# The last pass of an up projection on 64 rows: two token halves side by side in TensorE's array

## The chip, the cores and the metric

The kernel runs on one core of a Trainium2 chip. The metric is the device time of one execution in microseconds. One execution was also recorded by the hardware profiler; its rows are used below. PE is TensorE, DVE is VectorE, ACT is ScalarE, POOL is GpSimd and SP is SyncE. PEld is the part of TensorE that loads the stationary operand.

## What is computed

Three layers follow each other on x of 2 x 4160 tokens with 192 channels. The first is a softmax-weighted sum over 7 past tokens. The other two are these:

```python
xk = mu_k * x + (1 - mu_k) * x_prev          # layer 2, x_prev is the token before
k = np.maximum(xk @ w_k, 0.0)                # up projection 1: 192 -> 1024
v = k * k @ w_v                              # down projection 1: 1024 -> 192
r = 1 / (1 + np.exp(-(xr @ w_r)))            # xr is mixed with mu_r
x = r * v
h = np.maximum(x @ w_in, 0.0)                # layer 3, up projection 2: 192 -> 1024
gate = sigmoid(3-tap convolution of h over the tokens, per channel)
out = (h * gate) @ w_out                     # down projection 2
```

The change touches the two up projections alone. Both sum over 192 channels, that is 128 and 64 rows of the array.

## The kernel before, in words

**Tiles.** The 8320 tokens lie on 128 partitions with 65 tokens each. They are worked off in NG = 13 groups of G = 5, so that one group has N = 640 columns of tokens, in two halves of HN = 320. The 1024 hidden channels are NC = 8 chunks of 128.

**One chunk of an up projection** (up_products, L311 to L321) is written to a PSUM tensor of two banks, one half of the tokens in each. Each operand is split into a rounded part (hi) and a rest (lo) of type float32r. Five terms are summed, each for both halves, so a chunk has ten matmuls of 320 columns:

- terms 1 to 3 use the first 128 channels: w_hi with a_hi, w_lo with a_hi, w_hi with a_lo;
- terms 4 and 5 use the last 64 channels. Their tile a2 (xk2_s or y2_s) holds the hi part in one half of the partitions and the lo part in the other, and w2_hi and w2_lo hold the same 64 rows of weights twice. So term 4 gives w2_hi times (hi + lo) in one matmul, and term 5 gives w2_lo times (hi + lo).

For x the hi part of the last channels lies in partitions 0 to 63, for y in 64 to 127.

**Order on TensorE.** It is written out by hand. phase_a(i) (L431) holds the eight chunks of up1 for group i+1, the ten transposes of y of group i, the gate matmuls r_unit of group i+1, and the five blocks of down2 for group i-1. phase_b(i) (L444) holds the eight chunks of up2 for group i, the five blocks of down1 for group i+1 and the ten transposes of the attention result for group i+2. A loop runs both for i = 1 to 10. A chunk writes one of two PSUM tensors, up[c % 2]; from the third chunk on it waits until ACT has read the chunk two before (k_ok or h_ok).

**ScalarE.** k_relu (L546) and h_relu (L567) read a finished chunk out of PSUM. x_hi (L520 to L528) and y_hi_part (L530 to L540) make the hi parts; part 2 of either writes the 64 rows of a2. VectorE makes the lo parts from them (x_lo, L811; y_lo_part, L828).

**VectorE.** In phase_b(i) it works through six windows of convolution and gate (L843 to L857) of group i, and between them mixes x for group i+2 (L781 to L803) and multiplies y of group i+1 (y_mult, L818). The transposes of y that open the next phase_a wait for the last y_mult. In phase_a it ends the windows and computes the attention sum (L740, L745).

Of the kernel before, what the change touches and what calls it, by code (L numbers as in the profile page):

```python
# [25 lines left out]
F32R = mybir.dt.float32r  # L26
ALU = mybir.AluOpType
ACT = mybir.ActivationFunctionType
AX_X = mybir.AxisListType.X

P = 128


def mixer_kernel(nc, x, weight_gen, mu_k, mu_r, w_k, w_v, w_r, w_in, conv_w, w_out, out):
# [4 lines left out]
    NC = F // P  # L39
    D2 = D - P  # L40
# [3 lines left out]
    NG = TPP // G  # L44
    N = G * P
    HN = N // 2
# [4 lines left out]
    BANK = 512  # L51
# [18 lines left out]
    with ctx:  # L70
        def sb(name, shape, dt=F32):
            return ctx.enter_context(nc.sbuf_tensor(name, shape, dt))

        def sem(name):
            return ctx.enter_context(nc.semaphore(name))


        wk_hi, wk_lo, wk2_hi, wk2_lo = [sb(n, [P, F], F32R) for n in ("wk_hi", "wk_lo", "wk2_hi", "wk2_lo")]
        wi_hi, wi_lo, wi2_hi, wi2_lo = [sb(n, [P, F], F32R) for n in ("wi_hi", "wi_lo", "wi2_hi", "wi2_lo")]
# [21 lines left out]
        xkr2 = sb("xkr2", [P, N])  # L101
        xk_hi = sb("xk_hi", [P, N], F32R)
        xk_lo = sb("xk_lo", [P, N], F32R)
        xk2_s = sb("xk2_s", [P, N], F32R)
# [2 lines left out]
        y_hi = sb("y_hi", [P, N], F32R)  # L107
        y_lo = sb("y_lo", [P, N], F32R)
        y2_s = sb("y2_s", [P, N], F32R)
        HW = N + 5 * P  # L110
        h = sb("h", [P, NC * HW])
        cv = [sb(f"cv{i}", [P, N]) for i in range(2)]
# [3 lines left out]
        up = [ctx.enter_context(nc.psum_tensor(f"up{i}", [P, 2 * BANK], F32)) for i in range(2)]  # L116
        mid = ctx.enter_context(nc.psum_tensor("mid", [P, 2 * BANK], F32))
# [20 lines left out]
        x_used, at_step, at_sum, at_ok = [sem(n) for n in ("x_used", "at_step", "at_sum", "at_ok")]  # L138
        t_done, xt_ok, xt_free = [sem(n) for n in ("t_done", "xt_ok", "xt_free")]
        mix, xk_ok, xr_ok, x2_ok = [sem(n) for n in ("mix", "xk_ok", "xr_ok", "x2_ok")]  # L140
        xhi_ok, xlo_ok = sem("xhi_ok"), sem("xlo_ok")
        u1_done, k_ok, ksq_ok = [sem(n) for n in ("u1_done", "k_ok", "ksq_ok")]
        r_done, sg_ok, d_done, y_ok = [sem(n) for n in ("r_done", "sg_ok", "d_done", "y_ok")]
        yt_done, yhi_ok, ylo_ok = [sem(n) for n in ("yt_done", "yhi_ok", "ylo_ok")]
        u2_done, h_ok, h_free = [sem(n) for n in ("u2_done", "h_ok", "h_free")]
# [12 lines left out]
        def eq(g, n):  # L158
            return isinstance(g, int) and g == n
# [24 lines left out]
        def y_parts(g):  # L184

            return (xk_hi, xk_lo, xk2_s) if eq(g, NG - 1) else (y_hi, y_lo, y2_s)
# [64 lines left out]
        def _(pool):  # L251
# [16 lines left out]
            pool.wait_ge(h_ok, NC)  # L268
            nc.gpsimd.tensor_copy(h3[:, :, HW - 2 * P:HW], h3[:, :, 2 * P:4 * P]).then_inc(h_keep, 1)
            for g in range(3, NG):  # L270
# [4 lines left out]
        def _(pe):  # L275
# [32 lines left out]
                    pe.wait_ge(ylo_ok, 2 * g + 1)  # L308
                    transposes(mid, y, D, range(G), D2, yt_done)

            def up_products(dst, c, w_hi, w_lo, w2_hi, w2_lo, a_hi, a_lo, a2, done, part_ready):  # L311
                cols = slice(c * P, (c + 1) * P)
                terms = ((w_hi, a_hi), (w_lo, a_hi), (w_hi, a_lo), (w2_hi, a2), (w2_lo, a2))
                for t, (w, a) in enumerate(terms):
                    if part_ready is not None:
                        part_ready(t)
                    for half in range(2):
                        mm = nc.tensor.matmul(dst[:, half * BANK:half * BANK + HN], w[:, cols],  # L318
                                              a[:, half * HN:(half + 1) * HN],
                                              start=(t == 0), stop=(t == len(terms) - 1))  # L320
                mm.then_inc(done, 1)  # L321

            def up1(g, c):
                ready = None
                if c == 0:
                    def ready(t):
                        if t == 0:
                            pe.wait_ge(xhi_ok, 2 * g + 1)
                        elif t == 2:
                            pe.wait_ge(xlo_ok, 2 * g + 1)  # L330
                        elif t == 3:
                            pe.wait_ge(xhi_ok, 2 * g + 2)
                            pe.wait_ge(xlo_ok, 2 * g + 2)
                if c >= 2:
                    pe.wait_ge(k_ok, NC * g + c - 1)
                elif eq(g, 1):
                    pe.wait_ge(k_ok, NC - 1 + c)
                elif not eq(g, 0):
                    pe.wait_ge(h_ok, NC * g - NC - 1 + c)
                up_products(up[c % 2], c, wk_hi, wk_lo, wk2_hi, wk2_lo, xk_hi, xk_lo, xk2_s, u1_done, ready)  # L340

            def up2(g, c):
                ready = None
                if c == 0:
                    def ready(t):
                        if t == 0:
                            pe.wait_ge(yhi_ok, 2 * g + 1)
                        elif t == 2:
                            pe.wait_ge(ylo_ok, 2 * g + 1)
                        elif t == 3:  # L350
                            pe.wait_ge(yhi_ok, 2 * g + 2)
                            pe.wait_ge(ylo_ok, 2 * g + 2)
                if c >= 2:
                    pe.wait_ge(h_ok, NC * g + c - 1)
                elif eq(g, NG - 1):
                    pe.wait_ge(h_ok, NC * g - 1 + c)
                else:
                    pe.wait_ge(k_ok, NC * g + 2 * NC - 1 + c)
                up_products(up[c % 2], c, wi_hi, wi_lo, wi2_hi, wi2_lo, *y_parts(g), u2_done, ready)

            def r_unit(g, u):
                if u == 0:
# [13 lines left out]
            def down_block(dst, n, lhs, b, w, chunk_ready):  # L376
                for c in range(NC):
                    if chunk_ready is not None:
                        chunk_ready(c)
                    mm = nc.tensor.matmul(dst[:, n * D:(n + 1) * D], lhs[:, c, b * P:(b + 1) * P], w[:, c, :],  # L380
                                          start=(c == 0), stop=(c == NC - 1))
                return mm
# [48 lines left out]
            def phase_a(i, with_y=True, with_out=True):  # L431
                for c in range(NC):
                    up1(i + 1, c)
                    if with_y and c in (0, 2):
                        yt_part(i, c // 2 + 1)
                    if 3 <= c <= 5:
                        r_unit(i + 1, c - 3)
                    if with_out and c >= 5:
                        down2(i - 1, c - 5)
                if with_out:  # L440
                    down2(i - 1, G - 2)
                    down2(i - 1, G - 1)
# [51 lines left out]
            for n in range(2):  # L494
                def ready(c):
                    pe.wait_ge(g_ok, NC * NG + c + 1)
                mm = down_block(dn[0], n, gat3, n, wo_sb, ready if n == 0 else None)
# [4 lines left out]
        def _(act):  # L502
# [6 lines left out]
            def halves(v):  # L509
                return v.rearrange("p (s n) -> p s n", s=2)  # L510
# [9 lines left out]
            def x_hi(g, part):  # L520
                if part == 1:
                    if not eq(g, 0):
                        act.wait_ge(u1_done, NC * g)
                    act.wait_ge(xk_ok, g + 1)
                    nc.scalar.activation(xk_hi[:, :], xk1[:, :], ACT.Copy).then_inc(xhi_ok, 1)  # L525
                else:
                    act.wait_ge(x2_ok, g + 1)
                    nc.scalar.activation(xk2_s[0:D2, :], xkr2[0:D2, :], ACT.Copy).then_inc(xhi_ok, 1)  # L528

            def y_hi_part(g, part):  # L530
                hi, _, y2 = y_parts(g)
                act.wait_ge(yt_done, 2 * g + part)
                if part == 1:
                    if eq(g, NG - 1):
                        act.wait_ge(u1_done, NC * NG)
                    elif not eq(g, 0):
                        act.wait_ge(u2_done, NC * g)
                    nc.scalar.activation(hi[:, :], mid[:, 0:N], ACT.Copy).then_inc(yhi_ok, 1)
                else:
                    nc.scalar.activation(y2[D2:P, :], mid[D2:P, 0:N], ACT.Copy).then_inc(yhi_ok, 1)  # L540

            def k_relu(g, c):
                act.wait_ge(u1_done, NC * g + c + 1)
                if c == 0 and not eq(g, 0):
                    act.wait_ge(d_done, 3 * g)
                nc.scalar.activation(halves(ksq3[:, c, :]), up3[c % 2], ACT.Relu).then_inc(k_ok, 1)  # L546
# [10 lines left out]
                nc.scalar.activation(y[:, lo * D:hi * D], dn[u % 2][:, 0:(hi - lo) * D], ACT.Sigmoid).then_inc(sg_ok, 1)  # L557

            def h_relu(g, c):
                act.wait_ge(u2_done, NC * g + c + 1)  # L560
                if eq(g, 0):
                    pass
                else:
                    act.wait_ge(h_free, NC * g - NC + c + 1)
                    if eq(g, 1) and c == 0:
                        act.wait_ge(h_keep, 1)
                nc.scalar.activation(halves(h3[:, c, 2 * P:2 * P + N]), up3[c % 2], ACT.Relu).then_inc(h_ok, 1)  # L567
# [499 lines left out]
```

## Time and profile before

| | |
|---|---|
| median of 3 runs | 789.57 us (788.32 to 791.07) |
| span of the profiled execution | 788.2 us |
| its own time | not listed apart from the runs above; the fastest of them lies 0.1 us over the span, the median 1.4 us |
| PE busy | 731.6 us, 93% |
| PEld busy | 724.4 us, 92% |
| DVE busy | 653.0 us, 83% |
| ACT busy | 427.1 us, 54% |
| POOL busy | 11.8 us, 1% |

A row of a group of instructions shows the line, the engine, the operation, the tiles out<-in, the shape and the count, then the busy time and the mean duration of one. Matmuls overlap, so the busy time over the count is shorter than the mean duration: the first is the pace, the second the time from entering the array until the modelled end. "128*128" is the part of the array, rows by columns, that the instruction uses.

### The profile page before, as it was taken

How to read it: one execution, taken by the hardware profiler on the slowest of the kernel's cores; microseconds unless marked ns; L12 is line 12 of the kernel's file. 1: busy time of each engine (PE TensorE's matmuls, PEld its weight loads, DVE VectorE, ACT ScalarE, POOL GpSimd, SP SyncE). 2: the span in 40 equal slices, each digit the busy share in tenths (PEclk: the TensorE clock that was granted, in tenths of full speed). 3: DMA queues.
4: the chain of work that ended last, by engine and by line, in shares of the span. 5: the costliest groups of instructions: out<-in, count | busy, mean ns of one | idle time of the engine just before them, and what ended most of it. 6: DMA issues, size and time to landing. Idle time of an engine off the chain costs nothing.

```text
span 788.2 us, 12723 instructions
## 1 busy us (share of the span) xinstructions
PE 731.6 (93%) x4715; PEld 724.4 (92%) x4715; DVE 653.0 (83%) x834; ACT 427.1 (54%) x726; POOL 11.8 (1%) x21
## 2 busy tenths in 40 slices
PE   0199898999999999999999999999999999999898
PEld 0189898999999999999999999999999999999798
DVE  5898899799999899699697896996996996905794
ACT  1064746457457356366464473473563564655783
POOL 1000000000000000000000000000000000000000
PEclk9999999999999999999999999999999999999999
DMA  9501010020100200200200201102002000000001
GB/s 253 152 7 61 1 61 0 4 73 1 68 17 0 85 0 0 85 0 0 85 0 0 85 0 39 46 0 85 0 0 85 0 0 25 0 1 26 1 22 39
DMA packets 7831, 27.71 MB, mean 35 GB/s; under 512 B 940, under 2 KB 3716, under 8 KB 6274
## 3 DMA queue, kind: packets, MB, share of 16 engines
q1 hardware_dynamic: 7506, 26.39, 10.1%
q10 hardware_dynamic: 304, 1.05, 0.5%
q8 instruction: 12, 0.20, 0.1%
q14 instruction: 9, 0.07, 0.0%
HBM read 21.05 MB, written 6.39 MB: 35 GB/s over the span
## 4 chain that ended last, share of the span: by engine, by line
PE 49%; DVE 33%; issue 12%; ACT 3%; DMA 1%; DVEq 1%; SPq 0%; ACTq 0%
PE dn L380 23%; PE up L318 19%; DVE cv L846 8%; DVE gat L857 5%; DVE cv L843 4%; DVE prod L740 3%; PE dn L372 2%; PE dn L373 2%; DVE att L745 2%; PE mid L278 2%; DVE y L818 2%; DVE xk_s L811 1%; DMA xin<-in_x 1%; DVE cv L849 1%; ACT h L567 1%
## 5 line engine op out<-in xcount | busy, mean ns | idle before, releaser
L380 PE MATMUL dn<-wv_sb,ksq 128*128 128x192 f32 x1040 | 179.2, 326 | 0.0
L380 PEld LDWEIGHTS dn<-wv_sb,ksq 128*128 128x128 f32 x1040 | 169.7, 190 | 0.1
L380 PE MATMUL dn<-wo_sb,gat 128*128 128x192 f32 x992 | 167.0, 326 | 0.0
L380 PEld LDWEIGHTS dn<-wo_sb,gat 128*128 128x128 f32 x992 | 161.7, 190 | 0.0
L567 ACT ACTIVATE h<-up 128x640 f32<-128x640 f32 x104 | 73.1, 704 | 116.6 <-PE up L318 116.5
L546 ACT ACTIVATE ksq<-up 128x640 f32<-128x640 f32 x104 | 72.9, 701 | 67.6 <-PE up L318 65.7
L846 DVE SCALAR_TENSOR_TENSOR cv<-h,prm,cv 128x640 f32<-128x640 f32 x96 | 85.0, 886 | 26.9 <-ACT cv L590 23.8
L740 DVE TENSOR_TENSOR prod<-xin,wgt 128x960 f32<-128x960 f32 (+1 forms) x78 | 90.3, 1171 | 4.8
L843 DVE TENSOR_SCALAR cv<-h,prm 128x640 f32<-128x640 f32 x88 | 48.2, 548 | 55.3 <-ACT h L567 54.1
L745 DVE TENSOR_TENSOR att<-att,prod 128x960 f32<-128x960 f32 (+1 forms) x78 | 91.1, 1169 | 0.9
L572 ACT ACTIVATE cv<-cv 128x640 f32<-128x640 f32 (+1 forms) x100 | 72.2, 722 | 35.8 <-DVE cv L849 32.8
L849 DVE SCALAR_TENSOR_TENSOR cv<-h,prm,cv 128x640 f32<-128x640 f32 x96 | 86.5, 901 | 3.4
L857 DVE TENSOR_TENSOR gat<-h,cv 128x640 f32<-128x640 f32 x92 | 75.3, 819 | 0.3
L550 ACT ACTIVATE ksq<-ksq 128x640 f32<-128x640 f32 x104 | 74.9, 734 | 0.0
L318 PE MATMUL up<-xk_hi,wk_hi 128*128 128x320 f32 x208 | 57.4, 357 | 0.8 <-ACT xk_hi L525 0.8
L318 PE MATMUL up<-y_hi,wi_hi 128*128 128x320 f32 x192 | 52.7, 355 | 0.0
L318 PE MATMUL up<-xk_s,wk_hi 128*128 128x320 f32 x208 | 48.2, 313 | 2.5 <-DVE xk_s L811 2.5
L318 PE MATMUL up<-xk_lo,wk_hi 128*128 128x320 f32 x208 | 48.4, 314 | 0.0
L318 PE MATMUL up<-xk_hi,wk_lo 128*128 128x320 f32 x208 | 48.4, 314 | 0.0
L318 PE MATMUL up<-xk_s,wk_lo 128*128 128x320 f32 x208 | 47.9, 312 | 0.0
L601 ACT ACTIVATE o_sb<-dn 128x384 f32<-128x384 f32 (+1 forms) x39 | 16.9, 432 | 56.8 <-PE dn L380 56.8
L518 ACT ACTIVATE xt<-mid 128x640 f32<-128x640 f32 (+1 forms) x26 | 18.5, 712 | 53.3 <-PE mid L278 53.0
(119 smaller groups left out, 1112.2 us busy)
## 6 DMA issues: line engine op xcount, KB each, us to landing
xin<-in_x SPq DMA_DIRECT2D x11, 1152.0 KB, 5.4
out<-o_sb SPq DMA_DIRECT2D x12, 480.0 KB, 2.7
wgt<-in_weight_gen SPq DMA_DIRECT2D x1, 1680.0 KB, 12.0
xin<-in_x SPq DMA_DIRECT2D x1, 960.0 KB, 4.5
wv_sb<-in_moe_w_v SPq DMA_DIRECT2D x1, 768.0 KB, 12.8
wo_sb<-in_moe_w_out SPq DMA_DIRECT2D x1, 768.0 KB, 8.7
gat<-in_moe_w_k ACTq DMA_DIRECT2D x1, 512.0 KB, 4.9
gat<-in_moe_w_k ACTq DMA_DIRECT2D x2, 256.0 KB, 6.9
```

The source lines that it names most:

```text
L318: mm = nc.tensor.matmul(dst[:, half * BANK:half * BANK + HN], w[:, cols], a[:, half * HN:(half + 1) * HN], start=(t == 0), stop=(t == len( ...
L380: mm = nc.tensor.matmul(dst[:, n * D:(n + 1) * D], lhs[:, c, b * P:(b + 1) * P], w[:, c, :], start=(c == 0), stop=(c == NC - 1))
L546: nc.scalar.activation(halves(ksq3[:, c, :]), up3[c % 2], ACT.Relu).then_inc(k_ok, 1)
L550: nc.scalar.activation(ksq3[:, c, :], ksq3[:, c, :], ACT.Square).then_inc(ksq_ok, 1)
L567: nc.scalar.activation(halves(h3[:, c, 2 * P:2 * P + N]), up3[c % 2], ACT.Relu).then_inc(h_ok, 1)
L572: nc.scalar.activation(tile[:, 0:width], tile[:, 0:width], ACT.Sigmoid).then_inc(gs_ok, 1)
L740: nc.vector.tensor_tensor(v, x_tap(k), w_tap(k), ALU.mult)\
L745: nc.vector.tensor_tensor(acc, acc, term(k), ALU.add)\
L843: nc.vector.tensor_scalar(o[:, :], h3[:, c, P:P + N], taps[1], None, ALU.mult).then_inc(tap, 1)
L846: nc.vector.scalar_tensor_tensor(o[:, :], h3[:, c, 0:N], taps[0], o[:, :], ALU.mult, ALU.add).then_inc(tap, 1)
L849: nc.vector.scalar_tensor_tensor(o[:, :], h3[:, c, 2 * P:2 * P + N], taps[2], o[:, :], ALU.mult, ALU.add).then_inc(cv_ok, 1)
L857: nc.vector.tensor_tensor(dst[:, c, :], h3[:, c, P:P + N], conv_tile(w, c)[:, :], ALU.mult).then_inc(g_ok, 1)
```

## The change

Term 5 no longer takes all 128 rows. It multiplies w2_lo with the hi part alone, 64 rows, so the product of the two lo parts is left out. The lower half of the tokens runs in one half of the array's rows, the upper half of the tokens in the other half of the rows, each into its own bank. For that the hi part of one token half must also lie in the other 64 partitions: a new tile xy2_o takes it, by one more copy on ACT ahead of the old one in x_hi part 2 and in y_hi_part part 2. Each of the two last matmuls increments the semaphore, so the counts that ScalarE waits for are doubled.

```diff
+        xy2_o = sb("xy2_o", [P, HN], F32R)
...
-                terms = ((w_hi, a_hi), (w_lo, a_hi), (w_hi, a_lo), (w2_hi, a2), (w2_lo, a2))
+                terms = ((w_hi, a_hi), (w_lo, a_hi), (w_hi, a_lo), (w2_hi, a2))
...
                     for half in range(2):
                         mm = nc.tensor.matmul(dst[:, half * BANK:half * BANK + HN], w[:, cols],
                                               a[:, half * HN:(half + 1) * HN],
-                                              start=(t == 0), stop=(t == len(terms) - 1))
-                mm.then_inc(done, 1)
+                                              start=(t == 0), stop=False)
+
+                nc.tensor.matmul(dst[:, 0:HN], w2_lo[0:D2, cols], lower, start=False, stop=True).then_inc(done, 1)
+                nc.tensor.matmul(dst[:, BANK:BANK + HN], w2_lo[D2:P, cols], upper,
+                                 start=False, stop=True).then_inc(done, 1)
...
                             pe.wait_ge(xhi_ok, 2 * g + 2)
+                            pe.wait_ge(xo_ok, g + 1)
...
-                up_products(up[c % 2], c, wk_hi, wk_lo, wk2_hi, wk2_lo, xk_hi, xk_lo, xk2_s, u1_done, ready)
+                up_products(up[c % 2], c, wk_hi, wk_lo, wk2_hi, wk2_lo, xk_hi, xk_lo, xk2_s,
+                            xk2_s[0:D2, 0:HN], xy2_o[D2:P, :], u1_done, ready)
...
-                up_products(up[c % 2], c, wi_hi, wi_lo, wi2_hi, wi2_lo, *y_parts(g), u2_done, ready)
+                up_products(up[c % 2], c, wi_hi, wi_lo, wi2_hi, wi2_lo, *y_parts(g),
+                            xy2_o[0:D2, :], y_parts(g)[2][D2:P, HN:N], u2_done, ready)
...
                     act.wait_ge(x2_ok, g + 1)
+                    nc.scalar.activation(xy2_o[D2:P, :], xkr2[0:D2, HN:N], ACT.Copy).then_inc(xo_ok, 1)
                     nc.scalar.activation(xk2_s[0:D2, :], xkr2[0:D2, :], ACT.Copy).then_inc(xhi_ok, 1)
...
+                    if eq(g, NG - 1):
+                        act.wait_ge(u2_done, 2 * NC * g)
+                    nc.scalar.activation(xy2_o[0:D2, :], mid[D2:P, 0:HN], ACT.Copy).then_inc(yo_ok, 1)
                     nc.scalar.activation(y2[D2:P, :], mid[D2:P, 0:N], ACT.Copy).then_inc(yhi_ok, 1)
...
-                act.wait_ge(u1_done, NC * g + c + 1)
+                act.wait_ge(u1_done, 2 * (NC * g + c + 1))
...
-                act.wait_ge(u2_done, NC * g + c + 1)
+                act.wait_ge(u2_done, 2 * (NC * g + c + 1))
```

## Rows read from the trace of the kernel before

**Rows 1.** Stretches: length, busy time of PE, PEld, DVE, ACT, POOL, then PEclk.

```profile
0.00:75.96 75.96, 37.55 (x220) 35.72 (x221) 58.01 (x72) 25.41 (x36) 4.33 (x9) 1.00 0.43 122
75.96:129.00 53.04, 45.48 (x287) 44.69 (x287) 48.59 (x63) 30.48 (x49) 2.63 (x2) 0.96 0.07 23
129.00:683.49 554.49, 551.55 (x3596) 548.47 (x3596) 485.20 (x612) 307.03 (x525) 4.79 (x10) 1.00 0.08 28
683.49:738.00 54.51, 53.77 (x351) 53.49 (x350) 23.95 (x31) 32.02 (x55) 0.00 (x0) 1.00 0.03 10
738.00:788.20 50.20, 43.25 (x266) 42.01 (x266) 37.30 (x60) 32.13 (x64) 0.00 (x0) 1.00 0.07 25
```

**Rows 2.** The two stretches of one period, in the same columns.

```profile
435.01:461.13 26.12, 25.83 (x170) 25.53 (x170) 24.56 (x37) 13.57 (x23) 0.00 (x0) 1.00 0.17 63
461.13:490.42 29.29, 29.29 (x192) 29.29 (x193) 22.62 (x24) 16.43 (x30) 0.45 (x1) 1.00 0.00 1
```

**Rows 3.** The chain that ended last, pieces of that period: start, length, what.

```profile
433.53 1.48 PE up L318 x10
435.12 0.71 ACT h L567
435.95 0.56 DVE cv L843
...
459.91 0.82 DVE gat L857
460.73 0.28 DVE y L818
461.01 0.12 issue
461.13 0.76 PE mid L278 x5
461.89 0.15 PE up L318
```

**Rows 4.** Waits: engine and line, what for, us in total, times, longest.

```profile
PE mid L278 <- DVE y L818: 5.9, 10, 3.1
DVE cv L843 <- ACT h L567: 54.1, 9, 6.7
```

**Rows 5.** Groups of matmuls and of loads: busy us, mean ns of one.

```profile
L318 PE MATMUL up<-xk_s,wk_lo 128*128 128x320 f32 x208 | 47.9, 312 | 0.0
L318 PE MATMUL up<-y_s,wi_lo 128*128 128x320 f32 x192 | 43.9, 310 | 0.0
L318 PEld LDWEIGHTS up<-y_s,wi_lo 128*128 128x128 f32 x192 | 32.4, 189 | 0.0
```

**Rows 6.** Timeline inside a run of up chunks: start, busy length, engine.

```profile
403.20 0.46 PE L318 MATMUL up<-y_s,wi_hi 128*128 128x320 f32 x2
403.35 0.34 PEld L318 LDWEIGHTS up<-y_s,wi_lo 128*128 128x128 f32 x2
403.49 0.46 PE L318 MATMUL up<-y_s,wi_lo 128*128 128x320 f32 x2
403.79 0.45 PE L318 MATMUL up<-xk_hi,wk_hi 128*128 128x320 f32 x2
```

**Rows 7.** Timeline where the array had stood idle: two loads, their matmuls.

```profile
739.92 0.30 PEld L318 LDWEIGHTS up<-xk_s,wi_hi 128*128 128x128 f32 x2 [2.92 <-ACT xk_s L540]
```

**Rows 8.** Timeline of ACT and DVE around the second half of y.

```profile
411.12 0.70 ACT L540 ACTIVATE y_s<-mid 64x640 fp32r<-64x640 f32 x1
412.52 0.40 ACT L594 ACTIVATE h<-h 128x256 f32<-128x256 f32 x1
412.61 0.82 DVE L828 TENSOR_TENSOR y_s<-mid,y_s 64x640 fp32r<-64x640 f32 x1
```

**Rows 9.** Timeline of ACT and DVE around the second half of x.

```profile
41.38 0.74 ACT L528 ACTIVATE xk_s<-xkr 64x640 fp32r<-64x640 f32 x1 [1.58 <-DVE xkr L793]
42.15 0.82 DVE L811 TENSOR_TENSOR xk_s<-xkr,xk_s 64x640 fp32r<-64x640 f32 x1 [0.67 <-ACT xk_s L528]
...
451.42 0.72 ACT L528 ACTIVATE xk_s<-xkr 64x640 fp32r<-64x640 f32 x1
...
456.29 0.82 DVE L811 TENSOR_TENSOR xk_s<-xkr,xk_s 64x640 fp32r<-64x640 f32 x1
```

More of the change, by code:

```diff
@@ L140, in mixer_kernel @@
         mix, xk_ok, xr_ok, x2_ok = [sem(n) for n in ("mix", "xk_ok", "xr_ok", "x2_ok")]
-        xhi_ok, xlo_ok = sem("xhi_ok"), sem("xlo_ok")
+        xhi_ok, xlo_ok, xo_ok, yo_ok = [sem(n) for n in ("xhi_ok", "xlo_ok", "xo_ok", "yo_ok")]
         u1_done, k_ok, ksq_ok = [sem(n) for n in ("u1_done", "k_ok", "ksq_ok")]
@@ L309, in yt_part, with up_products @@
                     transposes(mid, y, D, range(G), D2, yt_done)
-            def up_products(dst, c, w_hi, w_lo, w2_hi, w2_lo, a_hi, a_lo, a2, done, part_ready):
+            def up_products(dst, c, w_hi, w_lo, w2_hi, w2_lo, a_hi, a_lo, a2, lower, upper, done, part_ready):
                 cols = slice(c * P, (c + 1) * P)
-                terms = ((w_hi, a_hi), (w_lo, a_hi), (w_hi, a_lo), (w2_hi, a2), (w2_lo, a2))
+                terms = ((w_hi, a_hi), (w_lo, a_hi), (w_hi, a_lo), (w2_hi, a2))
                 for t, (w, a) in enumerate(terms):
@@ L351, in ready @@
                             pe.wait_ge(yhi_ok, 2 * g + 2)
+                            pe.wait_ge(yo_ok, g + 1)
                             pe.wait_ge(ylo_ok, 2 * g + 2)
@@ L522, in x_hi @@
                     if not eq(g, 0):
-                        act.wait_ge(u1_done, NC * g)
+                        act.wait_ge(u1_done, 2 * NC * g)
                     act.wait_ge(xk_ok, g + 1)
@@ L534, in y_hi_part @@
                     if eq(g, NG - 1):
-                        act.wait_ge(u1_done, NC * NG)
+                        act.wait_ge(u1_done, 2 * NC * NG)
                     elif not eq(g, 0):
-                        act.wait_ge(u2_done, NC * g)
+                        act.wait_ge(u2_done, 2 * NC * g)
                     nc.scalar.activation(hi[:, :], mid[:, 0:N], ACT.Copy).then_inc(yhi_ok, 1)
                 else:
+                    if eq(g, NG - 1):
+                        act.wait_ge(u2_done, 2 * NC * g)
+                    nc.scalar.activation(xy2_o[0:D2, :], mid[D2:P, 0:HN], ACT.Copy).then_inc(yo_ok, 1)
                     nc.scalar.activation(y2[D2:P, :], mid[D2:P, 0:N], ACT.Copy).then_inc(yhi_ok, 1)
             def k_relu(g, c):
-                act.wait_ge(u1_done, NC * g + c + 1)
+                act.wait_ge(u1_done, 2 * (NC * g + c + 1))
                 if c == 0 and not eq(g, 0):
```

## The prediction

> **What bounds the kernel now.** I read the stretches of the span first. The loop of ten periods fills 129 to 683 us, and in it TensorE is busy 551.6 of 554.5 us at the full clock (PEclk 1.00, the upper of its two levels, 2.4 GHz), VectorE 485 and ScalarE 307 [rows 1]. So TensorE sets the pace of 70% of the span. But one period of 55.4 us has two parts, and the chain of waits shows that they differ [rows 2, 3]. From the transposes of y to the end of the first up2 chunk (29.3 us, the next phase A) the chain stays on TensorE, and VectorE has 6.7 us to spare ahead of its first window [rows 4]. From there to the last y_mult (26.1 us, phase B) the chain is VectorE's own, one instruction behind the other, 24.6 us busy; TensorE then stands for the last y_mult before it can transpose. The summed wait is 5.9 us in ten times, of which one, at the start, is 3.1, so about 0.3 a period [rows 4]; together with the issue of the first transpose I take 0.4. Phase B is thus held by two engines at once: a faster TensorE gains nothing there, a slower one costs all but those 0.4 us.
>
> Then the up chunks. Two 320-column matmuls of a term begin 0.29 us after the two before (403.20, 403.49, 403.79), so one enters every 147 ns, while each lasts about 308 ns by itself: a pair shows 0.455 us, less 0.147 [rows 6]; the group means are 310 and 312 [rows 5]. The array thus always holds two matmuls, the next one entering 161 ns (308 less 147) before the last one has left. A load starts with the matmul before its own and is hidden. Where the array stood idle, two loads show 0.30 us against 0.33 to 0.34 in the stream [rows 6, 7]; one load lasts 0.19 [rows 5], so a second load follows an idle start after about 0.11, which I take as what one load needs.
>
> **The change, part by part.** There are 13 x 8 x 2 = 208 chunks.
>
> Removed: two matmuls of 147 ns a chunk, 294 ns. Added: two matmuls of 64 rows, still 320 columns each. If they run beside each other they take the time of one, 147 ns, so the gain that is asked for is 147 ns a chunk.
>
> The change-over. Before, no matmul of 64 rows stands in the stream, so this price has no row and is bounded. In the eight matmuls ahead of the pair every result is the sum over all 128 rows; in the pair the lower and the upper rows must deliver separate sums to separate banks. With the old matmul still 161 ns inside, its last columns need the rows joined while the first of the pair need them apart. From below: nothing, as for the hand-over from one term to the next [rows 6], which changes only operands. From above, for the matmuls alone: each change-over lets the array empty, 161 ns, and there are two a chunk, into the pair and out of it. I take the upper value, because the reason why neighbours can overlap in rows 6 (all use the same joined rows) is the one the edit takes away, so the nearest row is that of one whole matmul, 308 ns. A chunk then costs 2 x 161 - 147 = 175 ns more.
>
> The Trainium skill states the same (TensorEngine Tiling (Array Packing), Key Properties: "Changing tiling mode (not just tile) drains the TensorE"). No run here shows it yet; it would also speak for the upper value.
>
> The two loads. The pair needs two loads as before. If the second begins only with the first of the pair, as each load begins with the matmul ahead of it now [rows 6], its matmul comes 108 ns late (0.30 less 0.19, rounded) and a chunk costs 283 ns more. If in addition neither load can run ahead of a change-over, two more loads of 108 ns lie open, 499 ns. I take none of these, since the two loads go to different rows, and keep both for the range.
>
> The copies. A copy of 256 columns takes 0.40 us and one of 640 takes 0.70 to 0.72, so one of 320 about 0.46 [rows 8, 9]; 26 of them are 12 us more on an engine that is busy 54%. In the loop the x half ends at 452.1 and its reader starts at 456.3, so 4 us cover it [rows 9]; without them the price would be 0.46 a period. The y half ends at 411.82 and its reader starts at 412.61: 0.79 against 0.46, still covered [rows 8]; what follows on ACT there is 0.46 later, and the next chunk's readers have waits to spare. At the start nothing covers it: VectorE waits for ACT and TensorE for VectorE (41.38, 42.15), 0.46 us [rows 9]. Near the end, for group 12, TensorE stands 2.9 us on the same two steps, 0.46 more [rows 7]. Together 0.9 us. The new semaphore waits belong to copies that are done before the lo parts, so nothing queues for them; the second increment costs nothing, since the reader waited for the later matmul before too.
>
> **The sum.** Of the 208 chunks, 80 lie in the phase A part of the ten periods, 16 in the start (first phase A and the one of 76 to 90 us) and 16 from 683 to 738 us, all in stretches where TensorE is busy end to end: 112. Another 80 lie in phase B of the ten periods, less 0.4 us a period. The remaining 16 (phase B of group 0, and up2 of group 12) stand among waits for VectorE and ScalarE (PE busy 45.5 of 53.0 us and 43.3 of 50.2 [rows 1]) and are costed at nothing; covered so, they would cost 2.8 us if that cover were gone. 192 x 0.175 = 33.6, less 10 x 0.4 = 4.0, plus 0.9: 30.5 us. On the profiled span of 788.2 that is 818.7. The median of the runs lies 1.4 us over this span, so the forecast is **820 us**.
>
> **The rivals.**
>
> (1) *Faster: no emptying.* The pair runs side by side and the change-over is free, as between terms. The gain is up to 147 ns a chunk; if the second load waits for the first of the pair, 108 ns late, it is 39. Phase B gives nothing, for VectorE holds it. 112 x 0.147 = 16.5 less 0.9 is 15.6: 774 us. With 39 ns: 4.4 less 0.9, 786 us. Middle: 780. For it: all hand-overs in the trace, between terms and between shapes, are seamless. Against it: none of them parts the rows. It decides from below 73 ns a change-over, half of 147.
>
> The skill (TensorE: Matmul & The Clock Gate, Part 3) tells of row tiles that start some 4 ns apart. That would bear out the 147 ns inside the pair; it says nothing of neighbours that use all rows, and no row here shows it.
>
> (2) *Same: the pair is not a pair.* The second of the 64-row matmuls follows the first after 147 ns, because of one stream of operands or of a load that needs as long in the stream as the matmul does (0.33 for two, 0.147 apart [rows 6]). Then ten matmuls stay ten, and with 0.9 us of copies it is 790.5 us. For it: a load and its matmul keep the same pace in the stream throughout. Against it: one load needs only 0.11 [rows 7].
>
> (3) *Much slower: the loads lie open too.* 192 x 0.283 - 3.1 is 51 us, 841; with 499 ns, 93 us, 882. It has the same sign as my forecast and fills the range upward.
>
> **How the numbers follow.** About 0.3% (2.4 us) is what a measurement here can tell from no change. Slower: 0.54, of which an incomplete emptying (some 795 to 815) 0.12, the forecast 0.24, open loads 0.18. Faster (rival 1): 0.33, some of it near 786. Same (rival 2, and gains and costs that cancel): 0.13. The range runs from 775, which leaves out only the perfect pair, to 862, half way between the two cases of open loads: about 0.08 below, 0.1 above. The likeliest case has 812 to 845 for itself.
>
> **What would show it.** By my forecast the profile after shows a period of 55.4 + 16 x 0.175 - 0.4 = 57.8 us; in a chunk the first matmul of 64 rows starts 0.31 us (not 0.147) after the last of 128 rows, the second within 0.02 us of it, and the next chunk's first 0.31 us after that. A chunk in a run of chunks takes 1.65 us, not 1.47. VectorE's wait for h grows in phase B. If the starts stand 0.147 apart all the way but the pair's two coincide, rival 1 is right, the chunk is 1.32 us and TensorE's wait for the last y_mult grows from 0.4 to about 1.6 us a period, so that only phase A shortens. If the pair's two matmuls are 0.147 apart, it is rival 2. The copies are wrong if TensorE waits for xy2_o in the loop. The forecast fails as a whole if the period stays at or under 55.4 us.

## The result and the profile after

The changed kernel takes 831.07 us (median of 4 runs, 830.75 to 832.39) against 789.65 us: slower by a ratio of 1.053, with a 95% interval of 1.0514 to 1.0546. The profiled execution spans 829.1 us, 40.9 more than the one before. The forecast was 820 us, with a range of 775 to 862.

The stretches of the span, for the same stages as in [rows 1], though not cut at exactly the same instructions. Columns: length, busy time of PE, PEld, DVE, ACT and POOL, PEclk, DMA share, GB/s.

```profile
0.00:79.30 79.30, 40.83 (x213) 35.45 (x214) 57.30 (x71) 25.80 (x37) 4.34 (x9) 1.00 0.40 117
79.30:134.60 55.30, 51.54 (x308) 44.52 (x306) 49.97 (x65) 32.92 (x53) 3.06 (x2) 0.97 0.07 22
134.60:718.53 583.93, 583.93 (x3575) 527.98 (x3575) 486.14 (x611) 314.27 (x543) 4.56 (x10) 1.00 0.07 26
718.53:771.00 52.47, 52.47 (x322) 47.96 (x320) 19.92 (x26) 27.88 (x48) 0.00 (x0) 1.00 0.03 10
771.00:829.10 58.10, 51.62 (x304) 46.98 (x302) 40.59 (x64) 38.84 (x74) 0.00 (x0) 0.97 0.06 21
```

VectorE does the same work as before; the clock is at its upper level in the loop, as it was before but for 3.4 us of the first period (127.9 to 131.3). What has changed is that TensorE shows no idle time at all in the loop, while its weight loads cover less of it.

In the start the clock differs as well. Two matmuls of 320 columns have a record of 0.73 us while the clock is at its lower level, and of 0.46 us at the upper one [rows 6]. The kernel before leaves the lower level at 46.0 us, the changed kernel at 50.9 (the PEclk column has no value for the time before that and shows 1.00):

```profile
45.39 0.73 PE L318 MATMUL up<-xk_lo,wk_hi 128*128 128x320 f32 x2
48.27 0.73 PE L321 MATMUL up<-xk_lo,wk_hi 128*128 128x320 f32 x2
```

The two parts of a period, to be held against [rows 2]:

```profile
455.76:483.44 27.68, 27.68 (x170) 24.83 (x171) 26.07 (x39) 13.91 (x24) 0.00 (x0) 1.00 0.16 57
483.44:514.53 31.09, 31.09 (x193) 28.29 (x192) 21.18 (x22) 17.02 (x32) 0.46 (x1) 1.00 0.01 3
```

A period is 58.77 us, not 55.42. Phase B grew by 1.56 us and phase A by 1.80. Now the chain of waits in phase B, which was VectorE's own in [rows 3], stays on TensorE (start, length, what):

```profile
478.57 1.17 PE up L321 x8
479.74 0.34 PE up L325
480.08 0.00 PE up L326
480.08 1.37 PE up L321 x8
481.45 0.34 PE up L325
481.79 0.00 PE up L326
481.80 1.37 PE up L321 x8
```

One chunk that follows another takes 1.37 + 0.34 = 1.71 to 1.72 us, where ten matmuls took 1.47: 0.248 us more, from the starts of single instructions. TensorE no longer stands for y_mult in the loop, and VectorE's wait for h has grown (from 6.7 in [rows 4], longest wait last):

```profile
PEld up L325 <- issue: 40.9, 208, 0.3
DVE cv L857 <- ACT h L581: 71.9, 10, 8.8
```

The first of these rows is new. In all 208 chunks the loading part of TensorE stands still ahead of the 64-row load, 40.9 / 208 = 0.197 us each. This is counted from the end of the load before, so it shows where TensorE stands and not yet what that costs. The timeline of one chunk shows where (start, busy length, engine):

```profile
430.08 0.46 PE L321 MATMUL up<-xk_s,wk_hi 128*128 128x320 f32 x2
430.46 0.18 PEld L325 LDWEIGHTS up<-xk_s,wk_lo 64*128 64x128 f32 x1 [0.19 <-issue]
430.46 0.41 PE L325 MATMUL up<-xk_s,wk_lo 64*128 64x320 f32 x1
430.46 0.18 PEld L326 LDWEIGHTS up<-xy_o,wk_lo 64*128 64x128 f32 x1
430.47 0.41 PE L326 MATMUL up<-xy_o,wk_lo 64*128 64x320 f32 x1
430.81 0.30 PEld L382 LDWEIGHTS dn<-wr_sb,xr 128*128 128x128 f32 x2 [0.16 <-issue]
430.81 0.59 PE L382 MATMUL dn<-wr_sb,xr 128*128 128x192 f32 x2
```

(L382 is the gate block that follows this chunk.) The last 128-row matmul starts 0.147 after 430.08, at 430.22. The 64-row load starts at 430.46: 0.24 later, or 0.09 beyond the slot of 0.147. It is not hidden either: the record of its matmul is 0.41 long instead of 0.31, because it waits 0.10 for its own weights. Both matmuls of the pair do start together, 3 to 4 ns apart in all 208 pairs. On the way out it is the same: the load for the next 128-row matmul starts at 430.81, 0.24 after the pair's real start at 430.57 (the start of its record and the 0.10 for the load), and its matmul waits 0.108 for it, seen from the next load (0.30 for two loads less 0.19). Each change-over thus costs 0.09 of standing still and 0.10 to 0.11 for an open load, some 0.198 us; two of them less the 0.147 that the pair saves are the 0.248 us. I call the 0.09 emptying. The record of the last 128-row matmul, whose end is modelled, lasts 0.31 us: the next matmul starts behind that end (0.345 after it), but its load starts before it (0.24), so what exactly the load waits for the trace does not show.

```profile
L325 PE MATMUL up<-xk_s,wk_lo 64*128 64x320 f32 x104 | 43.3, 417 | 0.0
L326 PE MATMUL up<-xy_o,wk_lo 64*128 64x320 f32 x104 | 43.3, 416 | 0.0
```

These are the groups in the place of L318 with wk_lo in [rows 5]: a mean of 417 ns instead of 312, the difference being the open load.

### The profile page after: what moved, and what is told of

It reads as the page before. It is cut to its first block, busy times and chain, and to the rows that moved or that the text cites. A ratio compares the mean times of both kernels' runs of the same rounds, so it can differ in the third digit from the quotient of the medians.

```text
span 829.1 us, 12750 instructions
## 1 busy us (share of the span) xinstructions
PE 780.4 (94%) x4715; PEld 702.9 (85%) x4715; DVE 653.9 (79%) x834; ACT 439.7 (53%) x752; POOL 12.0 (1%) x21
## 4 chain that ended last, share of the span: by engine, by line
PE 87%; DVE 8%; issue 2%; ACT 1%; DMA 1%; SPq 0%; DVEq 0%; ACTq 0%
PE dn L390 41%; PE up L321 29%; PE up L325 8%; PE mid L281 4%; PE dn L382 3%; PE dn L383 2%; DVE prod L754 2%; DVE att L759 1%; DMA xin<-in_x 1%; DVE cv L860 1%; DVE cv L857 1%; DVE gat L871 0%; DVE cv L863 0%; DVE wk_lo L959 0%; DVE att L754 0%
## 5 line engine op out<-in xcount | busy, mean ns | idle before, releaser
L390 PE MATMUL dn<-wv_sb,ksq 128*128 128x192 f32 x1040 | 185.4, 332 | 0.0
L390 PEld LDWEIGHTS dn<-wv_sb,ksq 128*128 128x128 f32 x1040 | 167.3, 190 | 9.6 <-issue 9.6
L390 PE MATMUL dn<-wo_sb,gat 128*128 128x192 f32 x992 | 169.6, 329 | 0.0
L860 DVE SCALAR_TENSOR_TENSOR cv<-h,prm,cv 128x640 f32<-128x640 f32 x96 | 84.9, 885 | 29.4 <-ACT cv L604 26.2
L863 DVE SCALAR_TENSOR_TENSOR cv<-h,prm,cv 128x640 f32<-128x640 f32 x96 | 84.9, 885 | 3.4
L321 PE MATMUL up<-xk_hi,wk_hi 128*128 128x320 f32 x208 | 60.6, 373 | 0.8 <-ACT xk_hi L535 0.8
L321 PE MATMUL up<-y_hi,wi_hi 128*128 128x320 f32 x192 | 55.1, 369 | 0.0
L528 ACT ACTIVATE xt<-mid 128x640 f32<-128x640 f32 (+1 forms) x26 | 18.5, 713 | 58.9 <-PE mid L281 58.8
L321 PE MATMUL up<-y_hi,wi_lo 128*128 128x320 f32 x192 | 44.1, 311 | 0.0
```

What stands on the lines that cost most here:

```text
L860: nc.vector.scalar_tensor_tensor(o[:, :], h3[:, c, 0:N], taps[0], o[:, :], ALU.mult, ALU.add).then_inc(tap, 1)
L863: nc.vector.scalar_tensor_tensor(o[:, :], h3[:, c, 2 * P:2 * P + N], taps[2], o[:, :], ALU.mult, ALU.add).then_inc(cv_ok, 1)
```

## The experiments

Nine kernels were run. The theory was the one just read: a change between 128-row and 64-row matmuls costs about 198 ns each way, and the pair itself is worth one slot. The rivals lay in the copies, in the 64-row matmuls themselves, in the number of rows, and in how much of a gain phase B would have let through.

**All but the matmuls.**

```diff
-                nc.tensor.matmul(dst[:, 0:HN], w2_lo[0:D2, cols], lower, start=False, stop=True).then_inc(done, 1)
-                nc.tensor.matmul(dst[:, BANK:BANK + HN], w2_lo[D2:P, cols], upper,
-                                 start=False, stop=True).then_inc(done, 1)
+                for half in range(2):
+                    nc.tensor.matmul(dst[:, half * BANK:half * BANK + HN], w2_lo[:, cols],
+                                     a2[:, half * HN:(half + 1) * HN],
+                                     start=False, stop=True).then_inc(done, 1)
```

> All of the change but its matmuls: the new tile, the 26 copies on ACT, the waits and the doubled increments, while term 5 stays two matmuls on all 128 rows. Theory (the cost is in TensorE's change-overs): 790.5 us, that is 0.9 over the kernel before, from the start and from group 12. Rival (the copies or the extra increments delay the readers of each chunk): a good part of the 41 us, over 800.

Measured 792.50 us, ratio 1.0037 (1.0023 to 1.0051) to a median of 789.32: 3.2 us, not 0.9. The rival is out, but the copies had been priced too low. The wait for the second half of x in the second group and the transposes of y behind it, before and in this kernel, then two more starts of these transposes:

```profile
74.43 0.54 PE L318 MATMUL up<-xk_s,wk_hi 128*128 128x320 f32 x2 [0.53 <-DVE xk_s L811]
75.19 0.76 PE L278 MATMUL mid<-ident,y 128*128 128x128 f32 x5
75.91 0.54 PE L321 MATMUL up<-xk_s,wk_hi 128*128 128x320 f32 x2 [1.02 <-DVE xk_s L826]
76.67 0.77 PE L281 MATMUL mid<-ident,y 128*128 128x128 f32 x5
463.35 0.65 PE L281 MATMUL mid<-ident,y 128*128 128x128 f32 x4 [0.29 <-DVE y L833]
518.85 0.76 PE L281 MATMUL mid<-ident,y 128*128 128x128 f32 x5 [0.28 <-DVE y L833]
```

The start has taken 1.5 us. The copy lies open twice in it, 0.49 us each time: for the first group, as was forecast, and again for the second, where the wait goes from 0.53 to 1.02. Of the other 0.5 us, 0.2 are a DMA that landed later, and the rest goes with a clock that left its lower level at 47.6 us instead of 46.0. The period is 55.50 against 55.42, 0.8 us over the ten, and the end is 0.5 us longer, as forecast. Why a period of which the copies are not on the chain is 0.08 longer was not followed up.

**Nine matmuls: the price of a free pair.**

```diff
-                    for half in range(2):
+                    for half in range(1 if t == 4 else 2):
...
-                                              start=(t == 0), stop=(t == len(terms) - 1))
+                                              start=(t == 0), stop=(t == (3 if half else 4)))
```

> The kernel before with the second matmul of term 5 left out (w2_lo is not applied to the upper token half), so nine matmuls of 128 rows a chunk: what a free pair would give. Theory (VectorE holds phase B, so that only 112 chunks pay): 789.7 less 112 x 0.147 = 773. Rival (all 208 chunks pay): 759.

Measured 780.50 us, ratio 0.9885 (0.9869 to 0.9902): 8.8 us less, neither 30.6 nor 16.5. The period is 54.64 us, 0.78 shorter, with these parts:

```profile
401.93:430.70 28.77, 28.64 (x185) 28.35 (x186) 22.63 (x24) 16.46 (x31) 0.45 (x1) 1.00 0.01 3
430.70:456.57 25.87, 24.42 (x161) 24.11 (x160) 24.55 (x37) 13.65 (x23) 0.00 (x0) 1.00 0.18 61
```

The cut at 430.70 lies 0.25 us further into its chunk than the one in [rows 2]; counted from the start of that chunk, phase A is 0.77 us shorter than before and phase B as long as before. Phase B is held as foretold: VectorE is busy 24.55 us there, as in [rows 2], and the wait for the last y_mult grows to about 1.5 us a period:

```profile
456.57 0.65 PE L278 MATMUL mid<-ident,y 128*128 128x128 f32 x4 [1.45 <-DVE y L818]
```

But phase A does not give its 8 x 0.147 = 1.18 us either. TensorE stands 0.4 us once a period ahead of down2. The sigmoid and the first load of down2, before and here:

```profile
416.37 0.50 ACT L557 ACTIVATE y<-dn 128x384 f32<-128x384 f32 x1
417.28 2.63 PEld L380 LDWEIGHTS dn<-wo_sb,gat 128*128 128x128 f32 x16
412.60 0.50 ACT L557 ACTIVATE y<-dn 128x384 f32<-128x384 f32 x1
413.23 0.95 PEld L380 LDWEIGHTS dn<-wo_sb,gat 128*128 128x128 f32 x6 [0.42 <-issue]
```

down2 takes a bank that ScalarE's sigmoid must have read (L410). The sigmoid ends at 413.10 and down2 follows at 413.23. Before, it ended at 416.87, 0.4 us ahead of the load. With TensorE faster, ScalarE's order of work in phase A is the next bound. The chunks of the start and the end gave less than their slots too: about 2 us, where 32 chunks at 0.147 had been counted as 4.7.

**One row half for both.** Both 64-row matmuls read the rows that hold the hi part; the sums stay those of the changed kernel.

```diff
...
-                nc.tensor.matmul(dst[:, 0:HN], w2_lo[0:D2, cols], lower, start=False, stop=True).then_inc(done, 1)
-                nc.tensor.matmul(dst[:, BANK:BANK + HN], w2_lo[D2:P, cols], upper,
+                nc.tensor.matmul(dst[:, 0:HN], w2_lo[rows, cols], lower, start=False, stop=True).then_inc(done, 1)
+                nc.tensor.matmul(dst[:, BANK:BANK + HN], w2_lo[rows, cols], upper,
...
-                            xk2_s[0:D2, 0:HN], xy2_o[D2:P, :], u1_done, ready)
+                            slice(0, D2), xk2_s[0:D2, 0:HN], xk2_s[0:D2, HN:N], u1_done, ready)
...
```

> The change with both matmuls of 64 rows in the same half of the rows, one token half after the other (the same sums as in the changed kernel). Theory (the pair in the changed kernel does run side by side, and the loss is in the two change-overs): one more slot of 147 ns in 192 chunks, 831 + 28 = 859 us. If the pair gained nothing from standing side by side: 831. If the price was that of two row halves being used together: near 790.

Measured 873.64 us (865.05 to 874.32), ratio 1.1031 (1.0973 to 1.1089). The period is 61.06 us, 2.29 more than in the changed kernel, or 16 x 0.143: the two follow each other, and the pair in the changed kernel did save its slot. Only the first of them pays for the open load:

```profile
L325 PE MATMUL up<-xk_s,wk_lo 64*128 64x320 f32 x104 | 43.8, 421 | 0.0
L326 PE MATMUL up<-xk_s,wk_lo 64*128 64x320 f32 x104 | 32.2, 310 | 0.0
```

It took 14.6 us more than the 859 that were expected, and most of that is a matter of the clock. The start is at the lower level until 59.0 us instead of 50.9, and the transposes of y first begin 5.2 us later than in the changed kernel, where eight more slots are 1.2. The other part lies near the end and is told in the last section.

**96 rows.**

```diff
+                    k = 96 if t == 4 else P
...
-                        mm = nc.tensor.matmul(dst[:, half * BANK:half * BANK + HN], w[:, cols],
-                                              a[:, half * HN:(half + 1) * HN],
+                        mm = nc.tensor.matmul(dst[:, half * BANK:half * BANK + HN], w[0:k, cols],
+                                              a[0:k, half * HN:(half + 1) * HN],
```

> The kernel before with term 5 on the first 96 of the 128 rows, for both token halves (part of the lo products and, for y, half of the hi products of w2_lo are left out). Theory (what counts is how the array is parted, and 96 rows leave it whole): 789.7 us, starts 147 ns apart. Rival (any change of the number of rows empties the array): ten slots and two change-overs of 198 ns, 192 x 0.396 less 4, about 861 us.

Measured 790.09 us, ratio 1.0008 (0.9998 to 1.0018). The group takes what it took with 128 rows (47.9 us and 312 ns in [rows 5]):

```profile
L319 PE MATMUL up<-xk_s,wk_lo 96*128 96x320 f32 x208 | 48.4, 314 | 0.0
```

So 96 rows among matmuls of 128 cost nothing. 96 rows are more than one half of the array and 64 are not; where between 64 and 96 the price begins was not tried.

**The two apart.**

```diff
...
+                        if t == 3 and half == 0:
+                            nc.tensor.matmul(dst[:, 0:HN], w2_lo[0:D2, cols], lower,
+                                             start=False, stop=True).then_inc(done, 1)
...
-                nc.tensor.matmul(dst[:, 0:HN], w2_lo[0:D2, cols], lower, start=False, stop=True).then_inc(done, 1)
```

> The changed kernel with its two matmuls of 64 rows apart: the one of the lower token half stands between the two matmuls of term 4, the other at the end. Four change-overs a chunk in place of two, and no pair. Theory (198 ns a change-over: 93 for emptying and 105 for a load that cannot run ahead): ten slots and four change-overs, 0.792 us more a chunk than before, 192 x 0.792 less 3, about 938 us. Rival (the price belongs to the 64-row matmuls themselves, not to the change of neighbours): no more than one slot over the changed kernel, 859.

Measured 952.40 us, ratio 1.2084 (1.2061 to 1.2106). The rival is out by 93 us; the theory's 938 was 14 us too low, again with a clock that stayed low longer, until 59.3 us at the start and for 27.3 us near the end. The period is 67.37 us, 11.95 over the kernel before; with the 0.4 us of cover that is 16 x 0.77, or 0.19 for each of the four change-overs. The loads stand still ahead of either:

```profile
PEld up L325 <- issue: 41.4, 208, 0.3
PEld up L328 <- issue: 33.7, 208, 0.3
```

**The pair twice.**

```diff
+                nc.tensor.matmul(dst[:, 0:HN], w2_lo[0:D2, cols], lower, start=False, stop=False)
+                nc.tensor.matmul(dst[:, BANK:BANK + HN], w2_lo[D2:P, cols], upper, start=False, stop=False)
```

> The changed kernel with the pair issued twice in a row (the product with w2_lo is added twice). Theory (two change-overs as before, and inside the 64-row part the loads run ahead again): one more slot of 147 ns in 192 chunks, 831 + 28 = 859 us. If loads stay open inside the 64-row part, 0.255 us a chunk: 880. If the second pair cannot overlap the first at all, 0.35 us a chunk: 898.

Measured 859.52 us, ratio 1.0896 (1.0878 to 1.0914), on the 859 of the theory. A second pair costs one slot, and its loads are hidden: the wait ahead of the first pair is 40.9 us as before, the second pair has none and the plain duration.

```profile
L326 PE MATMUL up<-xy_o,wk_lo 64*128 64x320 f32 x104 | 43.1, 415 | 0.0
L328 PE MATMUL up<-xy_o,wk_lo 64*128 64x320 f32 x104 | 32.0, 308 | 0.0
```

**Two pairs of neighbouring chunks side by side, and its control.** In phase A and phase B up(c) and up(c + 1) follow each other directly for even c, and what stood between them comes after. With pairs, the second chunk begins with its pair; the control has the same order and 128 rows throughout.

```diff
-                for c in range(NC):
-                    up1(i + 1, c)
...
+                for d in range(0, NC, 2):
+                    up1(i + 1, d)
+                    up1(i + 1, d + 1, True)
+                    for c in (d, d + 1):
...
+                if pair_first:
+                    nc.tensor.matmul(dst[:, 0:HN], w2_lo[0:D2, cols], lower, start=True, stop=False)
+                    nc.tensor.matmul(dst[:, BANK:BANK + HN], w2_lo[D2:P, cols], upper, start=True, stop=False)
```

> The changed kernel with two chunks brought together in phase A and phase B: the first ends with its pair, the second begins with its pair, so two pairs stand side by side and half of the change-overs go (all but the 16 chunks of up2 for groups 11 and 12). Theory (198 ns a change-over): a chunk costs 51 ns more than before, not 248. Phase B hides that in its 0.4 us, phase A does not: 789.7 + 104 x 0.051 + 8 x 0.248 + 0.9 is about 798 us. If the price were in the pairs, it would stay at 831.

> Control for the one with adjacent chunks: the kernel before with the same order of chunks, blocks and transposes, and all matmuls on 128 rows. Expected 789.7 us within 2 us by every theory; what it differs is the price of the order alone.

The control took 803.36 us (ratio 1.018, 1.0163 to 1.0197), so its expectation missed: the order costs 14.5 us by itself. With it the 798 us for the pairs missed as well. The second of two neighbouring chunks waits for ScalarE to empty its PSUM tensor:

```profile
PEld up L318 <- ACT ksq L550: 16.6, 24, 1.4
PE up L318 <- ACT ksq L550: 11.4, 12, 1.2
```

The kernel with pairs took 817.42 us (ratio 1.0368, 1.0351 to 1.0386), 14.1 over the control, where the change as it was made is 41.4 over its own. Per period it is 57.53 against 56.68 us, 0.85 or 16 x 0.053, and 51 ns a chunk were expected. The expectation had let phase B hide its half; here it does not, for in the control TensorE's wait for y_mult is already gone but for once (1.3 us). Half of the change-overs gone is most of the loss gone. Two pairs next to each other (start, busy length):

```profile
434.39 0.41 PE L332 MATMUL up<-xk_s,wk_lo 64*128 64x320 f32 x1
434.39 0.41 PE L333 MATMUL up<-xy_o,wk_lo 64*128 64x320 f32 x1
434.64 0.31 PE L318 MATMUL up<-xk_s,wk_lo 64*128 64x320 f32 x1
434.64 0.31 PE L319 MATMUL up<-xy_o,wk_lo 64*128 64x320 f32 x1
434.88 0.56 PE L324 MATMUL up<-xk_hi,wk_hi 128*128 128x320 f32 x2
```

**64 rows elsewhere.** The last test leaves the up projections alone and takes 64 rows in the gate blocks, in float32, without pair or copy.

```diff
-                    mm = nc.tensor.matmul(o, xkr2[:, b * P:(b + 1) * P], wr_sb[:, 1, :], start=False, stop=True)
+                    mm = nc.tensor.matmul(o, xkr2[D2:P, b * P:(b + 1) * P], wr_sb[D2:P, 1, :], start=False, stop=True)
```

> The kernel before with the second matmul of every gate block (r_unit, L373) on the 64 rows that hold its operand, in place of all 128 with zeros in the other 64; the sums are the same, the up projections are untouched. 65 blocks, each with a change-over in and one out. Theory (198 ns a change-over, for float32 as for float32r, with no pair and no copy about): 65 x 0.396 = 25.7 us in phase A, where TensorE sets the pace: about 815 us. Rival (the price belongs to two row halves used together or to the up chunks): 789.5.

Measured 813.36 us, ratio 1.0314 (1.0296 to 1.0333): 24.3 us for 65 blocks, 0.374 for the two change-overs of each. So neither a pair nor the copies are needed for the price. The zeros in the other 64 rows, which look like waste, are worth that much.

```profile
L373 PE MATMUL dn<-wr_sb,xkr 64*128 64x192 f32 x130 | 38.3, 375 | 0.0
PEld dn L373 <- issue: 14.6, 65, 0.2
```

No version tried beats the kernel before; only nine matmuls a chunk do, and they leave out a part that the others compute.

## Why the prediction was right, and where its terms were off

- **The bound.** Right. A slower TensorE costs in both phases; phase B gave back only the wait for y_mult, and the chain there moved from VectorE to TensorE. By the chunk's price the period should grow 16 x 0.248 less the 0.4 of cover, 3.6 us; it grew 3.35. The difference closes from the starts of the chunks. The cover was 0.51: before, the last chunk of the period takes 1.92 us (459.21 to 461.13) to the first load of the transposes and 0.06 more for that load, where a chunk takes 1.47. And the two chunks of a period that stand ahead of the transposes of y cost 0.05 less each, since the open load of a transpose is 0.06 long and not 0.11.
- **The pair.** Right: its two matmuls start together, and one row half for both costs 16 x 0.143 more a period. The Trainium skill (TensorE: Matmul & The Clock Gate, Part 3) lets matmuls on different row tiles start about 4 ns apart, and the trace agrees: 3 to 4 ns.
- **The change-over.** Right in kind, under-sized in amount; this is the term of the sum that failed. The Trainium skill (TensorEngine Tiling (Array Packing), Key Properties) says that a change of tiling mode drains TensorE. The trace above agrees as far as it reaches: the next matmul starts after the modelled end of the last one (0.345 against 0.31). The forecast took the whole remaining 161 ns for emptying and nothing for loads. Measured are 0.09 for emptying, since the next load starts 0.24 after the start of the last matmul and not 0.31, and 0.10 to 0.11 for a load that does not run ahead. The argument for leaving the loads out, that the two go to different rows, was wrong for what matters: they do not wait for each other, but the first load behind a change-over starts only 0.24 after the last matmul, whatever rows it goes to. 192 x (0.248 - 0.175) is 14 us too little.
- **The copies.** 0.9 was taken, 3.2 measured with all else as before. A copy of 320 columns took the 0.46 us that were taken (0.43 to 0.47), but at the start it lay open twice and not once, and the loop was not free.
- **The sum.** With both terms put right it would have been 30.5 + 14 + 2.3 = 47 us against 41.4 measured. The profiled spans, cut at the first transposes of y of each group, show where the rest went. The ten periods grew 32.4 us, not 160 x 0.248 - 4 = 35.7: 2.2 us by the 0.22 a period of the first point, and about 1 because the kernel before had its 3.4 us of low clock in the first of them. The start, up to these ten, grew 3.4 us, where 16 chunks and the copies come to 5.5: between 79 and 130 us nothing grew (50.97 us against 51.70), so the change-overs of the chunks that the forecast had counted there as open were covered, while the clock that stayed low until 50.9 us cost more (an estimate: half of 4.9, 2.4 us). The end grew 5.1 us. Errors of opposite sign, 16 us of terms put too low against 5 of cover put too low, made the forecast of 820 look closer than its parts were; that is luck.
- **Rival 1.** Out: the change-over is not free. Its price was wrong as well. The 16.5 us of gain would have been 8.8. A second bound, ScalarE's sigmoid ahead of down2, had only 0.4 us to spare and took 0.4 us of the gain in each period, and the chunks outside the ten periods gave about half of their slots.
- **Rivals 2 and 3.** The pair is a pair, and the second load does not wait for the first matmul. Open loads there are, but on top of a shorter emptying, so 0.248 a chunk and not 0.283 or 0.499.
- **The profile after.** Foretold were a period of 57.8 and a chunk of 1.65 us; they are 58.8 and 1.72.

## What to carry to other kernels

Before some matmuls of a stream are put on half of the rows, count the change-overs: here each costs 0.19 to 0.20 us, and a pair of 320 columns saves 0.147. By these numbers at least three pairs would have to stand together before the change pays; that is an estimate, and two were the most that was tried. Filling the idle rows of a matmul with zeros keeps the stream whole: in the gate blocks it is 24.3 us faster than leaving them out. Where two engines share the pace, price a gain by taking the work out for once: nine matmuls showed 8.8 us where the sum of slots said 30.6 and the best reading of the phases 16.5.

## What the runs showed that had not been expected

A matmul on 96 rows runs in the 128-row stream at the same pace, and one on 64 rows does not, alone or in a pair. The prediction had nothing on this; the theory behind the run had.

The load ahead of a change-over starts 0.24 us after the last matmul. In the kernel before, 4510 of the 4715 loads start within 5 ns of the start of a matmul.

The clock reached its upper level in the start at different times: at 46.0 us before and 50.9 in the changed kernel, at 59.0 and 59.3 in the kernels with one row half for both and with the two apart, but at 47.7 with the pair twice. Each kernel has the trace of one execution only, and no rule can be read from that.

Near the end of the kernels with one row half for both and with the two apart the granted clock fell to its lower level of 1.2 GHz for a long stretch: 23.9 us (from 813.4) in the one with one row half for both, 27.3 us (from 885.3) in the one with the two apart. It is the stage of up2 for the last group. In both TensorE had just stood 3.0 us for the lo part of y, which VectorE makes. Such a wait stands in the kernel before too [rows 7], without a fall of the clock, so it is not the cause by itself, and the cause stays open. The wait of the first kernel, then the stretches, first of the one, then of the other:

```profile
812.88 0.54 PE L321 MATMUL up<-xk_s,wi_hi 128*128 128x320 f32 x2 [2.99 <-DVE xk_s L843]
820.00:870.00 50.00, 49.05 (x244) 45.09 (x244) 31.25 (x52) 27.22 (x55) 0.00 (x0) 0.83 0.05 20
```

```profile
870.00:952.00 82.00, 72.35 (x334) 60.90 (x332) 44.31 (x69) 39.41 (x76) 0.00 (x0) 0.83 0.04 15
```

In the changed kernel PEclk is 0.97 in that stage. One of the four runs of the kernel with one row half took 865.05 us and the others 873.5 to 874.3. Its mean granted clock was 0.996 and that of the others 0.982 to 0.984; 23.9 us at half the clock are 0.014 of such a mean, so this is the run without the long stretch, and the stretch costs about 9 us.
